# Attention with one 132 wide block of probabilities a head: the scores of two key blocks merged in PSUM

## The reference, cut to what matters

```python
# attention: batch 4, 8 heads, 768 positions, head dim 64; n_sink = 4, window = 128
scores = q @ k.T / 8
keep = (key < 4) | ((pos - key >= 0) & (pos - key < 128))
a = softmax(where(keep, scores, -1e9)); x = a @ v          # [3072 tokens, 512]
# dense: d_ff = 2048
h = x @ w_in; x = (h - tanh(h)) @ w_out
# experts: 8, 1024 wide; one expert a token, by argmax of x @ w_gate + modality_bias
out = gate_w * (relu(x @ w1[e]) @ w2[e])
```

## Time and profile before

| what | value |
| --- | --- |
| median of 3 runs | 1071.74 us |
| the profiled execution's own time | 1070.08 us |
| its span | 1068.1 us |
| PE busy | 989.9 us (93%) |
| DVE busy | 650.4 us (61%) |
| ACT busy | 581.4 us (54%) |
| POOL busy | 327.3 us (31%) |
| chain that ended last | PE 73%, DVE 12%, ACT 6%, issue 5% |

### The profile page before, as it was taken

One profiled execution on the slowest core, in us unless ns is written; L12 is line 12 of the kernel. 1 busy time (PEld: TensorE's weight loads), 2 busy tenths in 40 slices (PEclk: granted clock), 3 DMA queues, 4 the chain that ended last, 5 costly groups with the idle time before them and its releaser, 6 DMA issues.

```text
span 1068.1 us, 23850 instructions
## 1 busy us (share of the span) xinstructions
PE 989.9 (93%) x7968; PEld 605.0 (57%) x7968; DVE 650.4 (61%) x2272; ACT 581.4 (54%) x1329; POOL 327.3 (31%) x462
## 2 busy tenths in 40 slices
PE   2748999999999999999999999999899999899996
PEld 1524444555554555555455556555487777677774
DVE  6665767667768767777866775646765334633331
ACT  4766786666667765766666675536422224522221
POOL 5766675112116211213511210101032232232322
PEclk9958999999999999999999999999999999999999
DMA  8710001201100320100210010041024211111111
GB/s 315 256 36 19 18 19 66 79 19 35 48 18 19 64 79 19 49 18 19 37 48 19 19 48 1 2 159 59 1 51 174 75 49 54 40 41 49 49 47 40
DMA packets 24375, 60.30 MB, mean 56 GB/s; under 512 B 9504, under 2 KB 9760, under 8 KB 22752
## 3 DMA queue, kind: packets, MB, share of 16 engines
q1 hardware_dynamic: 15392, 45.77, 13.2%
q0 software_dynamic: 5728, 13.43, 4.0%
q10 hardware_dynamic: 3168, 0.02, 0.1%
HBM read 45.35 MB, written 14.12 MB: 56 GB/s over the span
## 4 chain that ended last, share of the span: by engine, by line
PE 73%; DVE 12%; ACT 6%; issue 5%; POOL 1%; DVEq 1%; DMA 1%; ACTq 0%; SPq 0%; POOLq 0%
PE h_ps L751 19%; PE acc L807 18%; PE h_ps L1907 5%; PE s_ps L1856 5%; PE pt_ps L1856 5%; PE acc L1907 5%; PE pt_ps L639 4%; PE s_ps L569 3%; PE x_out L706 3%; ACT probs L587 2%; PE s_ps L858 1%; DVE qk_top L401 1%; PE pt_ps L662 1%; DVE pt_lo L648 1%; PE x_out L1833 1%
## 5 line engine op out<-in xcount | busy, mean ns | idle before, releaser
L807 PE MATMUL acc<-w_out_all,g_hi 128*128 128x512 f16 x768 | 228.4, 379 | 0.0
L751 PE MATMUL h_ps<-xt_hi,w_in_all 128*128 128x384 f16 x960 | 196.8, 328 | 4.2 <-DVE g_raw L772 3.0
L807 PE MATMUL acc<-w_out_all,g_lo 128*128 128x512 f16 x384 | 146.0, 380 | 3.3 <-DVE g_lo L792 2.7
L751 PEld LDWEIGHTS h_ps<-xt_hi,w_in_all 128*128 128x128 f16 x960 | 91.3, 100 | 62.3 <-issue 7.4
L807 PEld LDWEIGHTS acc<-w_out_all,g_hi 128*128 128x128 f16 x768 | 75.1, 98 | 77.7
L763 ACT ACTIVATE g_raw<-h_ps,batch_scale 128x384 f32<-128x384 f32 x120 | 69.5, 579 | 89.2 <-PE h_ps L751 85.3
L792 DVE SCALAR_TENSOR_TENSOR g_lo<-g_raw,batch_scale,g_hi 128x384 f16<-128x384 f32 x128 | 84.6, 661 | 44.4 <-ACT g_hi L782 44.4
L782 ACT ACTIVATE g_hi<-g_raw,batch_scale 128x384 f16<-128x384 f32 x128 | 77.9, 608 | 55.4 <-DVE g_raw L772 54.0
L101 POOL TENSOR_TENSOR tick<-tick 1x1 f32<-1x1 f32 x83 | 15.6, 188 | 293.4 <-ACT y L1923 116.2
L580 DVE CUSTOM_DVE_ANT_0 probs<-s_ps,mask 128x260 f32<-128x260 f32 (+1 forms) x192 | 70.0, 402 | 49.7 <-issue 43.9
L751 PE MATMUL h_ps<-xt_lo,w_in_all 128*128 128x384 f16 x480 | 98.3, 328 | 0.0
(11 more groups left out here) (315 smaller groups left out, 2098.2 us busy)
## 6 DMA issues: line engine op xcount, KB each, us to landing
qk_raw<-in_qk SPq DMA_DIRECT2D x31, 454.0 KB, 3.4
raw<-in_w SPq DMA_DIRECT2D x16, 512.0 KB, 8.1
v_raw<-in_v SPq DMA_DIRECT2D x4, 1536.0 KB, 7.0
x_tokens<-x SPq DMA_DIRECT2D x24, 256.0 KB, 2.5
w_in_all<-in_w_in SPq DMA_DIRECT2D x4, 1024.0 KB, 9.6
w_out_all<-in_w_out SPq DMA_DIRECT2D x4, 1024.0 KB, 9.0
x_tokens<-g_raw SPq DMA_DIRECT2D x1, 1024.0 KB, 12.7
vs_raw<-in_v SPq DMA_DIRECT2D x24, 4.0 KB
```

The lines of the kernel that those rows point to most:

```text
L751: mm = eng.matmul(h_of(m, f), w16[0][:, f, x * DM + k * P:x * DM + (k + 1) * P], r[:, par, k, :], start=(i == 0), stop=(i == 3 * KD - 1))
L807: mm = eng.matmul(acc[t][:, :], l[f % 2][:, t * P:(t + 1) * P], w16[1][:, f, x * DM:(x + 1) * DM], start=(f == 0 and i == 0), stop=(f == N ...
```

## The change

The block of 128 columns before and the own block are merged into one: where a column of the own block lies after the query (`past`), a predicated copy on DVE puts the score of the block before over it, in PSUM; a first pair gets -1e9 there. From there on a head has 132 columns (4 sinks and 128) in place of 260. After the transposition POOL parts the merged block again: one select writes the columns of the own block and zeros, another those of the block before and zeros, so that `weigh_values` reads what it read.

- DVE in `score_pair`: a predicated copy over both heads (for t = 1 of the first half of a batch also one over the sinks), a wait on its own semaphore `joined`, and a maximum over both heads read from PSUM; no sum is written to `probs`. The scale 1/8 goes into the scale of k (`SCALE_BITS`).
- ACT reads the scores from PSUM (132 wide, one instruction a head). PE's next scores wait for ACT's `exped` in place of DVE's `shifted`.
- `normalise`: one addition and one reciprocal for both heads; ACT's products are 132 wide.
- `transpose_probs`: 2 transposes for every pair; both halves are 256 wide and go to the new tile `merged`. POOL then runs two selects of 512 elements (one for a first pair), and PE's `weigh_values` waits for `parted`.
- `weight_split` of `w_in` (i = 0): DVE makes the low half in one instruction, one step after ACT's high half; POOL no longer touches these 16 parts. `w_out` stays as it is.

```diff
 def weight_split:
+    if E == "dve" and i == 0:
+        eng.wait_ge(q["w_hi0"], f + 1)
+        eng.scalar_tensor_tensor(lo, raw, w_scale[:, 0, 0:1], hi, ALU.mult, ALU.subtract).then_inc(q["w_lo0"], 1)
-    if E == "pool":
+    if E == "pool" and i == 1:
 def score_pair:
     pe:
-        claim_scores(eng, (q["shifted"], 2 * r + 1))
-        need(eng, q["shifted"], 2 * r)
+        claim_scores(eng, (q["exped"], 2 * r + 2))
+        need(eng, q["exped"], 2 * r)
     dve:
-        need(eng, q["normal"], 2 * (r - RING + 1))
-        eng.memset(tick[0:1, 4:5], 0.0)
-        for j in range(2):
-            eng.tensor_tensor_reduce(out=probs[:, r % RING, j, cols], in0=s_banks[j][:, cols], in1=m, scale=-SCALE, ...)
+        step(eng.copy_predicated(s_both[:, :, KB:KW], past[:, SINK:KB].unsqueeze(1).to_broadcast([P, 2, P]),
+                                 s_both[:, :, 0:P]))
+        eng.tensor_reduce(neg_max[:, r % RING, :], s_both[:, :, P:KW], AX.X, ALU.max, negate=True)
     act:
+        need(eng, q["normal"], 2 * (r - RING + 1))
         for j in range(2):
-            eng.activation(x, x, ACT.Exp, bias=neg_max[...], scale=-1.0, accum_out=...)
+            eng.activation(probs[:, r % RING, j, :], s_banks[j][:, P:KW], ACT.Exp, bias=neg_max[...], scale=1.0, accum_out=...)
 def normalise:
+        step(eng.tensor_scalar(totals, totals, 1e-9, DOWN, ALU.add, ALU.mult))
+        eng.reciprocal(totals, totals)
 def transpose_probs:
     pe:
-            for b in range(first, 2):
-                mm = eng.transpose(out[:, j, b - first, :], normed[:, 2 * t + j, b * KB:b * KB + P], ident[:])
+            mm = eng.transpose(out[:, j, :], normed[:, 2 * t + j, SINK:KB], ident[:])
     act and dve:
-        need(eng, q["pv_done"], free)
+        need(eng, q["parted"], parts(r - RING))
     pool:
+        eng.wait_ge(q["pt_lo_done"], m + 1)
+        need(eng, q["pv_done"], pv_count(TPC * (g - 1) + (1, 2, 2)[t]))
+        eng.affine_select(out=at[:, :, 1, :], in_=both, pattern=[[0, 4], [1, P]], compare_op=ALU.is_ge, fill=0.0, ...)
+        if not is_first(r):
+            eng.affine_select(out=at[:, :, 0, :], in_=both, pattern=[[0, 4], [-1, P]], compare_op=ALU.is_gt, fill=0.0, ...)
 def weigh_values:
-        eng.wait_ge(q["pt_lo_done"], turned(r) + (2 if last else 1))
+        eng.wait_ge(q["parted"], parts(r))
+        if last:
+            eng.wait_ge(q["pt_lo_done"], turned(r) + 2)
 def alone, turn r:
+        if E == "pool":
+            stage(transpose_probs, E, eng, r - 1)
 def window, slot k, behind before_slot and ahead of prepare and conversions:
+        if E == "pool" and even:
+            stage(transpose_probs, E, eng, ago(2))
```

More of the change, by code:

```diff
@@ L56 @@
 NEG = -1.0e9
-SCALE = float(D) ** -0.5
+SCALE_BITS = 3
+assert 4 ** SCALE_BITS == D
 ALONE = 14
@@ L159, in front @@
         payload = sb("payload", [P, TPC, 2], I32)
-        mask = sb("mask", [P, 3, KW], BF16)
+        later = sb("later", [P, KB], F32)
+        past = later[:].bitcast(I32)
+        never = sb("never", [P, 1], F32)
         ident = shared.ident
@@ L179, in front @@
         h_bank = ps("h_ps", [P, 512], F32)
-        s_banks = [ps(f"s_ps{j}", [P, 512], F32) for j in range(2)]
+        s_both = ps("s_ps", [P, 2, 512], F32)
+        s_banks = [s_both[:, j, :] for j in range(2)]
         s_bank = s_banks[0]
@@ L529, in sink_halves @@
                     eng.wait_ge(q["qk_mult"], 2 * (2 * HP * b + 1))
+                    eng.wait_ge(q["parted"], parts(max(r for at, r in scored.items() if at <= SLOTS * (2 * b - 2) + 22)))
                 eng.wait_ge(q["vs_hi_done"], b + 1)
@@ L546, in span, with joins, parts @@
             return slice(P if is_first(r) else 0, KW)
+        def joins(r):
+            return r + sum(i // PPC % 2 == 0 and i % TPC == 1 for i in range(r))
+        def parts(r):
+            return sum(1 if is_first(i) else 2 for i in range(r + 1))
         def pv_count(r):
@@ L576, in score_pair @@
+                eng.tensor_reduce(neg_max[:, r % RING, :], s_both[:, :, P:KW], AX.X, ALU.max, negate=True)\
+                   .then_inc(q["shifted"], 1)
+            if E == "act":
+                eng.wait_ge(q["shifted"], r + 1)
                 need(eng, q["normal"], 2 * (r - RING + 1))
[L577 to L578 removed]
                 for j in range(2):
[L580 to L582 removed]
@@ L590, in normalise @@
         def normalise(E, eng, r):
             a, t, hp, g = place(r)
[L593 to L607 removed]
+            totals = row_sum[:, r % RING, :, 0]
@@ new lines, in normalise @@
+            if E == "dve":
+                step = chain(eng, q["inverted"], 2 * r)
+                eng.wait_ge(q["exped"], 2 * r + 2)
+                step(eng.tensor_scalar(totals, totals, 1e-9, DOWN, ALU.add, ALU.mult))
+                eng.reciprocal(totals, totals).then_inc(q["inverted"], 1)
+            if E == "act":
+                eng.wait_ge(q["inverted"], 2 * r + 2)
+                need(eng, q["transposed"], turned(r) - TPC)
+                need(eng, q["sink_copied"], g)
+                for j in range(2):
+                    eng.activation(normed[:, 2 * t + j, :], probs[:, r % RING, j, :], ACT.Copy, scale=row_sum[:, r % RING, j, 0:1])\
@@ L625, in transpose_probs @@
             m = turned(r)
-            first = 1 if is_first(r) else 0
-            out = pt_bank[:].rearrange("p (j b c) -> p j b c", j=2, b=2)[:, :, first:2, :]
-            free = pv_count(TPC * (g - 1) + (1, 2, 2)[t])
-            def at(x):
-                return x[:, 0:12, :].rearrange("p (j t b) c -> p j t b c", j=2, t=TPC)[:, :, t, first:2, :]
+            out = pt_bank[:, 0:2 * P].rearrange("p (j c) -> p j c", j=2)
+            hi, lo = (merged[:, r % RING, x] for x in range(2))
             if E == "pe":
@@ L666, in transpose_sinks @@
                 need(eng, q["pv_done"], pv_count(TPC * g - 1))
-                eng.activation(pt_hi[:, 12:12 + TPC, :], out, ACT.Copy).then_inc(q["pt_hi_done"], 1)
+                eng.activation(pt_sinks, out, ACT.Copy).then_inc(q["pt_hi_done"], 1)
             if E == "dve":
                 eng.wait_ge(q["pt_hi_done"], m + 1)
-                low = pt_hi[0:STRIP, 12:12 + TPC, :]
+                low = pt_sinks[0:STRIP]
                 eng.tensor_tensor(low, out[0:STRIP], low, ALU.subtract).then_inc(q["pt_lo_done"], 1)
@@ L708, in weigh_values @@
                     mm = eng.matmul(x_out.rearrange("p (t c) -> p t c", t=TPC), vs_all[par][:, hp * P:(hp + 1) * P],
-                                    pt_hi[:, 12:12 + TPC, :], start=False, stop=True, skip_group_check=True)
+                                    pt_sinks, start=False, stop=True, skip_group_check=True)
                 mm.then_inc(q["pv_done"], 1)
```

103 lines of the change are left out of this document (48 added, 55 removed).

## The result

The changed kernel takes 1067.16 us (median of 6 runs, 1064.87 to 1068.55) against 1072.63 for the kernel before beside it: a ratio of 0.9942, 95% interval 0.9930 to 0.9954. It is faster, by 5.5 us and not by 20; 1051.5 was forecast, and 1067 lies outside the range. Its profiled execution took 1067.48 us, with a span of 1065.9.

A forecast was written before the change was run, and what follows sets the result against it. PE's own work was taken to bound the windows, waits between engines `alone`. -15.4 - 4 + 3 + 1 - 3.5 = -19 us on 1070.1 is 1051; forecast 1051.5, range 1043 to 1064.

The forecast's parts named there:

- PE's transposes: In the windows, two fewer transposes save 0.22 us of PE's flow in each of 70 full pairs: -15.4 us.
- `alone`, -3.5: The stretch up to the first dense matmul at 84.2 us gets 3.5 us shorter, between -9 and +4.
- the held banks: In `alone`, PE's next scores wait for ACT's exponentials, mostly beside DVE's inversion: 0 to +3 us.
- POOL's lateness at pair 9: In `alone`, k's low half starts late behind POOL's `w_in` parts; 2.9 us come free, less up to 1.28: -2.
- The sinks' waits, -4: In the windows, nine waits of the sink transposes for DVE's `pt_lo`, 8.1 us in all, lose 4 us.
- POOL in the windows: Selects hidden in most slots; +3 us where POOL is busy in window 0, +1 us for slot 25 in all windows.
- the slower rival: In the windows, POOL's selects come too late on every full pair and PE's products stall: near 1106 us; chance 0.06.
- `w_in` on DVE: 16 low halves at 0.79 us, 10 in `alone`, 6 in window 0 at no cost there; POOL loses 30 us.
- DVE and POOL stopping each other: Rival: POOL's selects and DVE's `g_lo` exclude each other in the windows, +12 us, 1063; chance 0.07.

The follow-up runs named there:

- e7: The changed kernel with DVE's four rank steps of slot 22 (windows 1 to 6) queued behind the sinks' gathering and merged low half: 1064.33 us, ratio 0.9915 to the kernel before.
- e12: The changed kernel with two score banks in turn and no selects or predicated copies for `alone`'s 14 pairs (attention left out): 1055.10 us, ratio 0.9841 to the kernel before.
- e1: The changed kernel with every second pair's scores in `alone` written to two other, idle PSUM banks: 1062.33 us, ratio 0.9910 to the kernel before.
- e3: The changed kernel without POOL's second select of a pair, except for pairs 1, 2 and 12 (result differs): 1062.70 us, ratio 0.9909 to the kernel before.
- e4: The kernel before with only `w_in`'s low halves moved to DVE, without the merge: 1072.09 us, ratio 0.9997 to the kernel before.
- e2: The changed kernel with all 16 low halves of `w_in` back on POOL, the merge kept: 1066.32 us, ratio 0.9941 to the kernel before.

## Why the prediction was wrong

At window 7 the forecast kernel would stand at 707.5 - 19 = 688.5 us; the changed one stands at 701.6, 13.1 late. By its steps:

- **PE's transposes**: right. 0.71 us a slot, and each full pair of windows 1 to 6 outside slots 20 to 26 is shorter by 0.22 or more: 58 x 0.22 = 12.8. The Trainium skill (TensorE: Matmul & The Clock Gate, Part 4: PE-mode transpose) gives about 275 ns for one 128 x 128 transpose inside a kernel. As the time of one instruction the traces agree (on the mean 284 ns before and 292 after, from 90 to 710 us); as a price of the flow, which by it would be 0.55 us for two, an estimate, they do not.
- **`alone`, -3.5**: the step that failed, +2.9, 6.4 us of the 13.1. I wrote of the held banks "the scores wait for ACT: 0.4 to 0.5 us of matmuls behind the exponentials, mostly beside DVE's inversion: 0 to +3" and took nothing for it in the -3.5, counted POOL's selects against one pair of `k_lo` and DVE's new pair of steps by its busy time alone. Shown instead: banks 2.0 us, selects 1.2, the copy 1.6 each by itself (2.7, 1.9 and 2.3 against e7), and 7.4 together (e12). Of the gains that I counted, POOL's lateness at pair 9 is gone:
```profile
57.27 0.52 ACT L448 ACTIVATE k_hi<-qk_raw 128x396 f16<-128x396 f32 x1
...
57.87 0.93 POOL L452 TENSOR_TENSOR k_lo<-qk_raw,k_hi 128x396 f16<-128x396 f32 x1 [3.08 <-ACT k_hi L448]
```
 But the high half itself stands 5.7 us later than in the earlier trace rows: the pairs ahead of it had lost that much. The clean error is one of kind: `alone` has no full engine, as I wrote, and yet I priced its parts by throughput. A chain through four engines is lengthened by latency.
- **The first slots of window 0**: another 1.4 us, by the granted clock. PE's is last but two in these rows, first the whole stretch in the changed kernel and its two parts, then the same two parts in e7:
```profile
87.10:99.40 12.30, 10.72 (x48) 4.61 (x49) 5.17 (x12) 4.23 (x11) 3.04 (x4) 0.63 0.13 38
87.10:96.10 9.00, 7.42 (x26) 2.93 (x26) 2.99 (x6) 1.70 (x3) 1.74 (x1) 0.50 0.17 52
96.20:99.30 3.10, 3.10 (x21) 1.58 (x22) 2.18 (x6) 2.43 (x8) 1.22 (x2) 1.00 0.00 0
...
87.80:91.60 3.80, 3.77 (x12) 1.64 (x12) 1.77 (x4) 0.53 (x1) 1.74 (x1) 0.50 0.14 12
91.70:98.40 6.70, 5.13 (x36) 2.58 (x36) 3.43 (x8) 3.66 (x10) 1.24 (x3) 1.00 0.16 61
```
 PE's clock is at its lower level, 0.50 (1.2 GHz), from 60 to 90 us with PE busy for 4.3 to 6.4 of every 10, and comes back in the first dense slots: 9.0 us after the first dense matmul in the changed kernel, 3.8 in e7 with the same code up to there, 4.5 in the kernel before. The whole stretch had a mean of 0.63, of 0.79 before (84.2 to 95.1 us) and of 0.83 in e1; e7 took 10.6 us for it, less than the 10.9 before. So nothing ties these 1.4 us to the merge: e3 has them too, and so has e4, which doesn't merge.
- **The sinks' waits, -4**: failed, 8.9 for 8.1. I shortened the path from PE over ACT to DVE's low half, but DVE itself was the late one, before the change as after it: the wait has the name of the last instruction, and the queue ahead of that one is not in it. I priced the path by the wait's total, without the row of what DVE did in the 2 us before; what stood in that queue was not to get shorter. With the further waits in slots 20 to 26 that is 4.6 us in windows 1 to 6 (-11.2 in place of -15.8), of which 1.0 is window 2's scatter.
- **POOL in the windows**: right. 1.9 us of waits, the select as priced; the slower rival stayed far off. Window 0 came out at +1.06 where the forecast has +3 - 12 x 0.22 = +0.4; the stretch from 139 to 167 us did not get shorter. The missing 0.7 is less than what DVE's low halves of `w_in` cost there (next point).
- **`w_in` on DVE**: put at nothing in window 0, since DVE has 30% idle there; it costs 1.1 us in slots 2 to 12 without the merge (e4 against before) and 0.9 in slots 2 to 9 with it (changed against e2). Its worth was put at 3 us of `k_lo`; up to the first dense matmul it is 0.9 without the merge and 4.4 with it, and at the end neither shows in the ratios.
- **DVE and POOL stopping each other**: rows of it are there, and small. A step on three columns, 0.17 us before the change (L894 there), beside a select:
```profile
244.12 0.63 POOL L662 TENSOR_SCALAR_AFFINE_SELECT pt<-merged 128x512 f16<-128x512 f16 x1 [0.51 <-DVE merged L656]
244.17 0.61 DVE L914 TENSOR_SCALAR den<-den 128x3 f32<-128x3 f32 x1
...
250.94 0.63 POOL L662 TENSOR_SCALAR_AFFINE_SELECT pt<-merged 128x512 f16<-128x512 f16 x1 [0.45 <-DVE merged L656]
250.99 0.62 DVE L944 TENSOR_TENSOR work<-work,chosen 128x24 f32<-128x24 f32 x1
```
 The second step, with two SBUF inputs, takes 0.62 us here and 0.18 at the least. The Trainium skill (SBUF — State Buffer, SBUF: two separate sides) states that a VectorE instruction in a 2-port mode or with two SBUF inputs and a GpSimd instruction that reads SBUF exclude each other for the whole instruction. The second pair of rows agrees; the first fits only by the 2-port mode, which the prediction left out and the trace doesn't name. PE's time hardly feels it: e3, with nearly every second select gone, shows no gain in the windows that is clear of scatter.

The four shortfalls, 6.4 + 1.4 + 4.6 in windows 1 to 6 + 0.7 in window 0, are the 13.1 us; 2.4 of them, as said, come and go between executions. Of what would make the forecast wrong, it had named "if `alone` gets longer": it did.

## What to carry to other kernels

Where no engine is full, price a change by latency: how long from this input to the first output that someone waits for, and how long each buffer is held now. Two heads joined in one instruction save an engine's time and delay the first head. A wait is priced only with the waited-for engine's queue in front of it; if that has no gap, a shorter path to it gives nothing, and reordering it moves part of the wait (0.49 us of 0.74 stayed won in three windows). And causes on one chain are tested together as well as one by one, and read at more than one place: up to the first dense matmul 2.0, 1.2 and 1.6 us were 7.4, but by the ratios of the whole runs 3.4, 6.7 and 4.6 us were 10.8, less than their sum. So whether they strengthen each other is not shown.

## What was not expected of the hardware

A predicated copy of 128 x 256 in PSUM, with mask, source and destination, takes 428 ns, 15 more than a plain subtraction of that width (413). A select of 128 x 512 two-byte elements on POOL takes 666 on the mean. Beside such a select, a DVE step of 24 columns that takes 0.18 us at the least took 0.62. Two executions with the same code up to there had the granted clock back at 1.00 at 9.0 and at 3.8 us behind the first dense matmul. The stretch from slot 2 of window 7 on, the same instructions in all fourteen profiles, takes 360.5 to 364.5 us: a gain under 4 us can't be read from one pair of spans, only from stage starts or medians.
